# Gram products of two scan steps issued together, with batches moved to a neighbouring quadrant in half of the steps

## What is computed

```python
k_n = k / (norm(k) + 1e-06)
for t in range(768):                      # state: 4 x 8 matrices of 48 x 48
    y[t]  = q[t] @ state
    state = state + beta[t] * outer(k_n[t], v[t] - k_n[t] @ state)
a, b = x @ w1, x @ w2                     # x: 3072 x 384, w1 and w2: 384 x 1024
x = (a * b) @ w3 @ w_out
logits = x @ phi                          # 3072 x 32
slot_input = softmax(logits, over tokens).T @ x
slot_out[e] = relu(slot_input[e] @ w1[e]) @ w2[e]          # 8 experts, 4 slots each
out = softmax(logits, over slots) @ slot_out
```

## Time and profile before

| | before |
|---|---|
| median of 3 runs | 498.75 us |
| profiled execution: its time | 501.24 us |
| profiled execution: span of the core | 499.3 us |
| PE busy | 461.0 us, 92% of the span (9921 matmul passes) |
| DVE, ACT, POOL busy | 242.5, 227.9, 185.1 us |
| chain that ended last, by engine | PE 75%, POOL 6%, DVE 5%, DMA 5%, issue 4% |
| chain, costliest lines | L1189 34%, L1091 4%, L1125 4%, L1106 4%, L1140 3%, L1075 4% |

### The profile page before, as it was taken

One profiled execution on the slowest core, in us unless ns is written; L12 is line 12 of the kernel. 1 busy time (PEld: TensorE's weight loads), 2 busy tenths in 40 slices (PEclk: granted clock), 3 DMA queues, 4 the chain that ended last, 5 costly groups with the idle time before them and its releaser, 6 DMA issues.

```text
span 499.3 us, 21733 instructions
## 1 busy us (share of the span) xinstructions
PE 461.0 (92%) x9921; PEld 334.9 (67%) x9921; DVE 242.5 (49%) x499; ACT 227.9 (46%) x408; POOL 185.1 (37%) x329
## 2 busy tenths in 40 slices
PE   5586899999999899999999999999999999999982
PEld 5435467877778677777777777776777777754442
DVE  3899576356453656345284253834342332144123
ACT  1134455545546454555444654554554553324112
POOL 1001499811688315883038860188800000000000
PEclk9998999999999999999999999999999999999997
DMA  8999004320014400054000442000080085699949
GB/s 221 385 266 368 1 4 97 89 76 5 3 47 86 127 4 5 2 129 129 5 3 3 96 95 71 4 4 3 3 328 13 3 321 189 214 413 427 421 176 372
DMA packets 21979, 64.98 MB, mean 130 GB/s; under 512 B 2048, under 2 KB 7552, under 8 KB 20736
## 3 DMA queue, kind: packets, MB, share of 16 engines
q1 hardware_dynamic: 21440, 62.81, 37.0%
q10 hardware_dynamic: 448, 0.79, 0.6%
HBM read 58.87 MB, written 4.72 MB: 127 GB/s over the span
## 4 chain that ended last, share of the span: by engine, by line
PE 75%; POOL 6%; DVE 5%; DMA 5%; issue 4%; ACT 1%; SPq 1%; DVEq 0%; POOLq 0%
PE pA L1189 17%; PE pB L1189 17%; PE pKY L1091 4%; PE pD L1125 4%; PE pKY L1106 4%; PE pKY L1140 3%; DMA step_slab<-e_dram 3%; POOL prep_slab L473 3%; POOL prod_p L472 3%; PE pT L1205 3%; PE pG L1205 2%; PE pG L1075 2%; PE pT L1075 2%; PE pD L1213 2%; DMA arena<-kq_dram 2%
## 5 line engine op out<-in xcount | busy, mean ns | idle before, releaser
L730 DVE TENSOR_TENSOR arena<-a_sb,pB 128x512 f32<-128x512 f32 x41 | 28.2, 687 | 130.1 <-PE pB L1189 130.0
L472 POOL TENSOR_TENSOR prod_p<-prep_slab 128x30 f32<-128x30 f32 (+9 forms) x150 | 75.2, 501 | 43.2 <-DVE prep_slab L796 32.2
L473 POOL TENSOR_TENSOR prep_slab<-prep_slab,prod_p 128x30 f32<-128x30 f32 (+9 forms) x150 | 82.3, 549 | 11.8
L512 ACT ACTIVATE step_slab<-pKY 32x384 f32<-32x384 f32 x92 | 44.4, 483 | 35.9 <-PE pKY L1140 34.2
L1189 PE MATMUL pB<-whi,xhi 128*128 128x512 f32 x135 | 55.9, 414 | 0.0
L1189 PE MATMUL pB<-whi,xlo 128*128 128x512 f32 x135 | 53.2, 394 | 0.0
L1189 PE MATMUL pB<-wlo,xhi 128*128 128x512 f32 x135 | 52.7, 391 | 0.0
L1189 PE MATMUL pA<-whi,xhi 128*128 128x512 f32 x135 | 51.9, 439 | 0.0
L1189 PE MATMUL pA<-whi,xlo 128*128 128x512 f32 x135 | 47.2, 400 | 0.2
L1189 PE MATMUL pA<-wlo,xhi 128*128 128x512 f32 x135 | 45.6, 393 | 0.0
L453 POOL TENSOR_TENSOR arena<-arena,nrm 128x1152 f32<-128x1152 f32 (+1 forms) x11 | 17.9, 1630 | 48.9 <-DVE prep_slab L818 48.2
(11 more groups left out here) (290 smaller groups left out, 877.6 us busy)
## 6 DMA issues: line engine op xcount, KB each, us to landing
arena<-e_dram SPq DMA_DIRECT2D x7, 1536.0 KB, 14.6
arena<-kq_dram SPq DMA_DIRECT2D x44, 192.0 KB, 5.8
arena<-kv_dram SPq DMA_DIRECT2D x16, 384.0 KB, 4.9
late_w<-e_dram SPq DMA_DIRECT2D x4, 1536.0 KB, 9.7
arena<-w3t_dram SPq DMA_DIRECT2D x2, 2048.0 KB, 19.4
arena<-w_dram SPq DMA_DIRECT2D x1, 4096.0 KB, 14.1
out_dram<-late_w SPq DMA_DIRECT2D x6, 576.0 KB, 5.4
arena<-kv_dram SPq DMA_DIRECT2D x2, 1536.0 KB, 19.7
```

The source lines that it names most:

```text
L472: link(nc.gpsimd.tensor_tensor(pv, a, x, ALU.mult))
L473: link(nc.gpsimd.tensor_tensor(dst, dst, pv, ALU.add))
L512: nc.scalar.activation(xs[q, :], pKY[q, bank(g, b), 0:DM], ACT.Copy).then_inc(y_done, 1)
L730: nc.vector.tensor_tensor(ab_tile(s, p)[:, half * HF:(half + 1) * HF], a_sb[:], up_bank(t, half, 1), ALU.mult).then_inc(ab_done, 1)
```

## The change

1. **Quadrants.** In the scan steps s = 2 and 3 of each iteration batch b lies in quadrant b ^ 1 (`quarter`). The loads of keys and values put the two later steps' rows there, and `solve_rows`, `state_step`, `y_step`, `y_out` and `key_merge` follow. The output tokens of a batch now always stand in its own quadrant.
2. **Grams.** `grams` takes a pair of scan steps, (0, 2) or (1, 3), and half of the heads. A burst is again 32 products. For one head it now holds the four batches of both steps, which lie on eight different parts of the array, in two banks of PSUM. Both steps of a pair count as done at the end of its second burst.
3. **Place of the bursts (n > 1).** Before, all four stood among the first two groups of `up`. Now the first pair stands among the first group, and the second pair among the third group, behind `state_step` and `ab_turn`. VectorE masks the second pair behind `state`; ScalarE copies it out behind `abt_out(t, 0)`. For n = 1 the bursts stay ahead of `state_step`, with the second burst three products later.
4. **Order elsewhere.** ScalarE runs `a_out(t, 0)` ahead of the first `gram_out`. For n = 1, `scale` and `turn_back` of step s = 3 stand behind `ab_mul` of half 1, not ahead of it.
5. **Loads.** Beta comes in eight pieces of 16 partitions (12 KB each), which are issued behind both pieces of w3; `set_up(0)` waits at its head for all eight. Keys and values come in five pieces per iteration (before: one for iterations 0 and 1, four afterwards).
6. **Removed.** The three groups of 32 products at L1258, L1263 and L1268. The 47 products at L1241 write another bank.

```diff
@@ gpsimd and sync helpers
 def landed(k):
-    return 16 + 64 * k
+    return 80 * (k + 1)
+        GRAM_ORDER = [0, 2, 1, 3]
+        def quarter(g, b):
+            return b ^ (g % STEPS // 2)
+        def quad(x):
+            return slice(32 * x, 32 * x + 32)
@@ sync, before the loop
                 sp.dma_start(*kq_piece(0, 0, i, 0)).then_inc(kq_first[i], 16)
-            sp.dma_start(beta_sb[:], beta).then_inc(beta_in, 16)
             sp.dma_start(phi_sb[:], phi.rearrange("(c p) f -> p c f", p=128)).then_inc(phi_in, 16)
             sp.dma_start(wot_raw, wot.rearrange("(c p) f -> p c f", p=128)).then_inc(wot_in, 16)
             load_w3t(0)
             load_w3t(1)
+            for b in range(B):
+                for s in (0, STEPS // 2):
+                    q = 32 * quarter(s, b) + H * s
+                    sp.dma_start(beta_sb[q:q + 2 * H], beta[32 * b + H * s:32 * b + H * s + 2 * H]).then_inc(beta_in, 16)
             reload_kq(1, 1)
@@ scalar, body
+                    a_out(t, 0)
                     gram_out_at(0)
-                    a_out(t, 0)
                     gram_out_at(1)
                     z_out(g)
...
-                    gram_out_at(2)
-                    gram_out_at(3)
+                    if n == 1:
+                        gram_out_at(2)
+                        gram_out_at(3)
...
                     abt_out(t, ts, 0)
+                    if n > 1:
+                        gram_out_at(2)
+                        gram_out_at(3)
@@ vector, set_up and body
                 if is_first(n):
-                    dve.wait_ge(beta_in, 16)
+                    dve.wait_ge(beta_in, 16 * 2 * B)
...
                         mask_at(0)
                         mask_at(1)
-                        mask_at(2)
                     ab_mul(t, ts, 0, tp)
                     if n == 1:
                         mask_at(2)
+                        mask_at(3)
...
-                    mask_at(3)
                     if g < NT - 1:
                         state(g)
+                    if n != 1:
+                        mask_at(2)
+                        mask_at(3)
...
-                    if s == 3 and fin and prep:
+                    if s == 3 and fin and prep and n > 1:
                         scale(n + 1)
                         turn_back(n + 1, q)
                     ab_mul(t, ts, 1, tp)
+                    if s == 3 and n == 1:
+                        scale(n + 1)
+                        turn_back(n + 1, q)
@@ tensor, grams
-            def grams(n, p, k, s, t):
+            def grams(n, p, k, pair, half, t):
+                if half == 0:
+                    for r in range(2):
+                        pe.wait_ge(kq_in[p][r], keys_landed(p, k))
+                    if pair > 0:
+                        pe.wait_ge(gs_done, n * STEPS + 2)
+                        if n > 2:
+                            pe.wait_ge(abt_done, t * 2 + 1)
+                    else:
+                        pe.wait_ge(abt_done, t * 2)
+                        pe.wait_ge(xlo_done, t)
                 apart(pe, pe_passed)
-                gram_products(p, s, GRAM_BANKS[s % 2])
+                gram_products(p, pair, GRAM_BANKS, half * H // 2, half * H // 2 + H // 2)
+            def gram_products(p, pair, banks, h0=0, h1=H):
                 for h in range(h0, h1):
+                    for i, s in enumerate(GRAM_ORDER[2 * pair:2 * pair + 2]):
+                        for b in range(B):
+                            r = 64 * (b % 2)
+                            last = mm(banks[i][quad(quarter(s, b)), h * 64:h * 64 + 64],
+                                      KQ[p][r:r + D, b // 2, h, 0, C * s:C * s + C],
+                                      KQ[p][r:r + D, b // 2, h, :, C * s:C * s + C], start=True, stop=True)
@@ tensor, body, s == 0 and prep, n > 1
-                        up(t, 0, 0, None, 0, 8)
-                        grams(n + 1, q, k1, 0, t)
-                        up(t, 0, 0, None, 8)
-                        grams(n + 1, q, k1, 1, t)
+                        up(t, 0, 0, None, 0, 5)
+                        grams(n + 1, q, k1, 0, 0, t)
+                        up(t, 0, 0, None, 5)
+                        grams(n + 1, q, k1, 0, 1, t)
+                        up(t, 0, 1, None, 0, 2)
                         solve_rows(g, p, s, n)
-                        up(t, 0, 1, None, 0, 6)
-                        grams(n + 1, q, k1, 2, t)
-                        up(t, 0, 1, None, 6)
-                        grams(n + 1, q, k1, 3, t)
+                        up(t, 0, 1, None, 2)
...
                     if g < NT - 1:
                         state_step(g, p, k, s, n)
-                    ab_turn(t, ts, tp, 0, made - 1 if s == 0 and prep else had)
+                    ab_turn(t, ts, tp, 0, had + 2 if s == 0 and prep else had)
+                    if s == 0 and prep:
+                        up(t, 1, 0, None, 0, 4)
+                        grams(n + 1, q, k1, 1, 0, t)
+                        up(t, 1, 0, None, 4, 8)
+                        grams(n + 1, q, k1, 1, 1, t)
+                        up(t, 1, 0, None, 8)
+                        up(t, 1, 1, None, 0, 3)
+                        y_step(g, p, s)
+                        up(t, 1, 1, None, 3)
```

128 lines of the change are left out of this document (55 added, 73 removed).

## The result

The changed kernel takes 522.47 us (median of four runs, 521.78 to 524.24) beside 498.57 for the kernel before on the same chip: a ratio of 1.0487 with a 95% interval of 1.0454 to 1.0521. It is 24 us slower; 12 were forecast. The profiled execution has a span of 520.2 us, 20.9 more than before. The profiled execution of the kernel before was itself 2.7 us above its median, so some 3 of the 24 us do not show when the two profiles are compared.

A forecast was written before the change was run, and what follows sets the result against it. TensorE, busy 92% of the span, was taken as the bound, with VectorE's chain at the start and in step 12. Start +10.4, step 4 -1.4 and steps 8 to 16 +2.95 made +11.95: 510.7 us, range 502 to 515 (own range 507 to 514.5).

The forecast's parts named there:

- Beta: At the start, beta behind w3 is complete at 28.0, delaying VectorE 13.0 us and `solve_rows` of step 0 by 10.4 us.
- a little tail behind it for eight small pieces: At the start, beta's pieces land shortly behind w3's second piece, so beta is complete between 26.8 and 28.9.
- The seven further issues: On SyncE's queue at the start, beta's extra issues take 4.1 us, hidden behind the wait for beta and put at nothing.
- rival 1: At the start, small pieces overtake w3, beta is not late and `solve_rows` starts at 48.9: 496.6 us; chance 0.13.
- A burst on eight parts: In the gram bursts, issue falls from 0.86 to 0.45 us: -0.41 us a burst, -1.64 for a step's four.
- Rival 3: Eight parts gain nothing at full clock because issue limits the bursts, which keep 0.86 us: 517.0 us; chance 0.05.
- Step 4: For n = 1, bursts give -1.64 us and completing the pair before masks and `r_rows` costs 0.2: -1.4 us.
- Steps 8, 12 and 16: For n = 2 to 4, VectorE's chain sets the end and the bursts' gain does not arrive: +2.95 us in all.
- The place of the last burst: In steps 8, 12 and 16 the last burst ends 13.2 us after the step's start, against 11.70 before.
- Idle gaps of TensorE that no engine ends are taken as equal in both: In steps 8 to 16, such gaps (0.89 us in step 12) were assumed the same before and after the change.
- The waits in steps 9, 13 and 17: `ab_turn` of the second half waits for `ab_mul`, 2 to 4 us in all with the wait for `xlo`.
- Rival 2: In steps 8 to 16 the bursts' gain arrives too, -1.64 us each, if VectorE's chain keeps clear: 502.9 us; chance 0.16.

The follow-up runs named there:

- e4_before_beta_late: The kernel before, with its single transfer of beta issued behind both pieces of w3: 512.36 us, ratio 1.0261.
- e1_beta_first: The changed kernel with its eight pieces of beta issued ahead of phi, not behind w3: 510.02 us, ratio 1.0191 to the kernel before.
- e2_old_places: e1_beta_first with the bursts of steps 8, 12 and 16 at their places of before, still on eight parts: 499.99 us, ratio 1.0004 to the kernel before.

## Why the prediction was wrong

The direction was right, and 522.5 lies above the range's end of 515. The forecast's two mechanisms are both in the trace; each was sized too small, one assumption was false, and the clock in the loop had no term. The forecast's own range was also added up too narrow: its bounds give 505.8 to 515.1, not 507 to 514.5, which changes nothing here.

**Beta.** The wait at `set_up`'s head, the work queued behind it and the way to `solve_rows` came as written. From `set_up(0)` to L732's start it is 29.29 us against 29.28 before, and the three products took 5.28 us at 0.50 (forecast 5.2). The term that failed is "a little tail behind it for eight small pieces": beta was complete at 31.1, not 28.0, and past the upper end of 28.9. This end had been set by w3's own landing, as if small pieces could only be fast. Seven of the eight did land ahead of w3 (26.3 to 28.9), so the order of landing is not that of issue, which the prediction had as unshown; but the wait is for all eight, and the last, issued at 20.6, came 1.9 us behind w3. The seven further issues were put at nothing. With one transfer (e4_before_beta_late) it is 28.57, within the bounds. That `solve_rows` starts there at 63.05, the forecast's very number, is luck: beta is 0.6 later than forecast and the three products 0.6 shorter. At step 1 it is 11.1 us; the 2.5 us between the two kernels come on top and make the +13.6, where 10.4 were forecast.

**Beta not late (rival 1).** The forecast for this case was a `solve_rows` at 48.9. In e1_beta_first it is at 50.1. The argument that 384 fewer instructions end TensorE's idle stretch before 43.7 was wrong: it is 5.27 us long there and ends at 45.02, as a block of instructions ends it, not the amount of work. And the 2.6 us that were won were lost again by step 1, 1.7 of them to the clock and 0.65 to the stall inside `solve_rows`.

**A burst on eight parts.** Forecast 0.41 us less, measured 0.23. The step that failed read 14 to 15 ns a pass, in products that ran at half rate, as the array's own rate and halved it. (That this was half clock it took from the passes' times; the granted clock of the earlier trace rows reads 1.00 at 20 to 22 us.) At full clock the 64 passes and the change to the next tile take 0.79 us. Rival 3 (no gain at all) is refuted by the same rows.

**Step 4.** Forecast -1.4, measured +0.7. The bursts gave back 4 x 0.23 = 0.9. Against that stand three stretches without a releaser of 0.74, 0.62 and 0.15 us, where the kernel before has 0.20, which is 1.3 us more. The 0.3 that is left has no row of its own.

**Steps 8, 12 and 16.** Forecast +2.95 in all, measured +8.6. That `set_up` would start late and that the next step would wait for `ab_mul` and `xlo` is what the rows show; from `set_up` to the end of `xlo` it is 9.47 us in step 12 (forecast 9.5), and masks and copies take 1.68 (forecast 1.8). Counted as the forecast counts, from the start of the step to the third triple, the three steps measured 26.92, 26.19 and 27.07 us, where 26.4, 24.5 and 24.5 were forecast: 7.65 more than before. The other 1.0 lies behind that point. Three terms failed.
- *The place of the last burst.* Its successor was forecast for 13.2 us after the step and came at 14.99 in step 12. By the rows of both kernels, the four bursts gave back 1.3 and not 1.64; the eight more products of `up`, now in six groups instead of four, took 2.6 and not 1.84; and `solve_rows` took 1.44 us to the next work where it took 0.81, of which 0.36 is the idle stretch at 258.21.
- *The clock.* Nothing in the sum stood for it. The third triple took 1.53 us in step 9 and 1.34 in step 13, not 0.90, and in step 17 it started 0.3 after `xlo` was done, because the triples before it ran at 0.50. That is 1.3 to 1.4 us in all.
- *The idle stretches.* In step 16 a stall of 1.16 us fell inside the fourth burst, on VectorE's chain; `set_up` starts 17.26 us after that step, 0.6 later than in step 12. "Idle gaps of TensorE that no engine ends are taken as equal in both" is the assumption that was false. They are where blocks of instructions begin; with other counts ahead they fall elsewhere, and when they fall ahead of the last burst they delay that chain.

That step 8 comes out so near its forecast (26.92 and 26.4) is luck: its `set_up` is late by the first term too, but only 0.7 us later than in step 12, not the 1.9 of the forecast. The waits in steps 9, 13 and 17 make 5.9 us, not 2 to 4. Rival 2 (the bursts' gain arrives there) is refuted.

**Taken together**, these stretches measured 22.9 us where 11.95 were forecast, and the miss of 11 is 3.2 at the start, 2.1 in step 4 and 5.7 in steps 8 to 16. e1_beta_first gives back the first and e2_old_places the last, and both together return the kernel to the time of before, without the eight parts' gain.

## What to carry to other kernels

A small transfer that a head-of-queue wait needs goes ahead of the large ones, and its wait goes down to the first use: here 12.5 us and 5.0 us. Before bursts are moved later in a step, follow what the other engine has queued behind them up to the next wait, and count from the end of the last burst, since a shorter burst at a later place is late. Read the granted clock behind every new wait: the 2 us waits here cost their own length and up to 0.6 us more. Look at the count of instructions ahead of the first critical products as at a resource: with 32 unneeded tiny products at the start the kernel before became 7 us slower and e2_old_places 4 to 5, and 2 to 4 us of that show ahead of step 1.
